# First pair of heads: the products of q and k ahead of the decay's matmuls, and the scaled decay sum behind the low part

## The reference, cut to what matters

```
scores = scale * q @ k.T                         # 32 heads of 576 x 64
cum    = cumsum(log(clip(f, 1e-4, 1)))           # one row of 576 for each head
decay  = cum[:, None] - cum[None, :]
scores = where(causal, -1e9, scores + decay)
attn   = softmax(scores);  y = attn @ v
x      = y of all heads, 2304 tokens x 512
h      = relu(x @ w_in)**2 @ w_out               # 512 -> 2048 -> 512
out    = the same with a quadratic-then-linear gate and a second pair of weights
```

## Time and profile before

| | |
|---|---|
| median of 3 runs | 948.94 us (948.78 to 949.65) |
| the profiled execution | 948.56 us |
| its span, first to last instruction | 946.7 us |
| TensorE busy | 938.7 us, 99% |
| VectorE, ScalarE, GpSimd busy | 65%, 68%, 18% |
| granted clock of TensorE | 1.00 throughout |

### The profile page before, as it was taken

The page is one execution under the profiler, slowest core; times in us unless marked ns, Lnnn a source line. Parts: engine busy times, 40 slices in busy tenths (PEclk is TensorE's granted clock), DMA queues, the critical chain, the costliest instruction groups (busy, mean ns, idle before and its releaser), DMA issues.

```text
span 946.7 us, 16672 instructions
## 1 busy us (share of the span) xinstructions
PE 938.7 (99%) x5554; PEld 865.6 (91%) x5554; DVE 613.5 (65%) x1279; ACT 642.2 (68%) x1342; POOL 167.8 (18%) x217
## 2 busy tenths in 40 slices
PE   8999999999999999999999999999999999999998
PEld 8999999989999999999999999898989888888897
DVE  7888888786666543446353588878766565755454
ACT  7888888886667655557564587666766566756564
POOL 7877999910000000000000000000000000000000
PEclk9999999999999999999999999999999999999999
DMA  6546555075557525252525144646545434364401
GB/s 217 168 152 181 162 190 159 24 245 176 191 187 290 200 101 187 114 197 104 200 102 201 45 153 141 239 133 262 228 179 193 174 132 169 130 229 143 165 24 68
DMA packets 61942, 155.13 MB, mean 164 GB/s; under 512 B 4624, under 2 KB 28688, under 8 KB 61872
## 3 DMA queue, kind: packets, MB, share of 16 engines
q1 hardware_dynamic: 61872, 154.23, 46.4%
HBM read 120.06 MB, written 34.15 MB: 163 GB/s over the span
## 4 chain that ended last, share of the span: by engine, by line
PE 96%; POOL 2%; issue 1%; ACT 1%; DVE 0%; POOLq 0%; ACTq 0%; DVEq 0%
PE banks L1469 37%; PE banks L1515 21%; PE banks L1507 14%; PE banks L1509 7%; PE banks L1413 6%; PE banks L1358 5%; PE banks L1368 4%; PE banks L1426 1%; PE banks L1384 1%; POOL wi_raw L780 1%; PE banks L1417 0%; PE banks L1409 0%; ACT pr L868 0%; POOL qk L692 0%; POOL xs L835 0%
## 5 line engine op out<-in xcount | busy, mean ns | idle before, releaser
L1469 PE MATMUL banks<-xs,wi_hi 128*128 128x384 f32 x1344 | 342.4, 335 | 1.4 <-ACT s_tile L942 0.7
L1469 PEld LDWEIGHTS banks<-xs,wi_hi 128*128 128x128 f32 x1344 | 235.2, 188 | 22.0 <-issue 1.9
L1469 PE MATMUL banks<-xs,wi_lo 128*128 128x384 f32 x672 | 224.7, 334 | 0.0
L1515 PE MATMUL banks<-wo_hi,gs 128*128 128x512 f32 x576 | 202.3, 393 | 0.0
L1507 PE MATMUL banks<-gs,wo_hi 128*128 128x512 f32 x384 | 141.7, 391 | 0.3 <-issue 0.3
L966 ACT ACTIVATE gs<-h_tile 128x384 fp32r<-128x384 f32 x192 | 100.7, 525 | 52.7 <-DVE h_tile L1214 50.0
L1469 PEld LDWEIGHTS banks<-xs,wi_lo 128*128 128x128 f32 x672 | 126.2, 188 | 0.0
L1515 PEld LDWEIGHTS banks<-wo_hi,gs 128*128 128x128 f32 x576 | 108.1, 188 | 18.8 <-DVE gs L1219 0.2
L942 ACT ACTIVATE s_tile<-banks 128x384 f32<-128x384 f32 x144 | 70.1, 487 | 76.3 <-PE banks L1469 76.1
L1515 PE MATMUL banks<-wo_lo,gs 128*128 128x512 f32 x288 | 113.7, 395 | 0.0
L1219 DVE TENSOR_TENSOR gs<-h_tile,gs 128x384 fp32r<-128x384 f32 x192 | 106.3, 554 | 7.0 <-ACT gs L966 6.1
(11 more groups left out here) (112 smaller groups left out, 1465.7 us busy)
## 6 DMA issues: line engine op xcount, KB each, us to landing
wi_hi<-kept_weights SPq DMA_DIRECT2D x32, 896.0 KB, 5.7
wi_lo<-kept_weights SPq DMA_DIRECT2D x32, 896.0 KB, 7.9
wo_raw<-moe_w_out_dram SPq DMA_DIRECT2D x48, 512.0 KB, 3.9
kept_weights<-wi_hi SPq DMA_DIRECT2D x16, 896.0 KB, 6.3
kept_weights<-wi_lo SPq DMA_DIRECT2D x16, 896.0 KB, 8.1
qk_raw<-qk_dram SPq DMA_DIRECT2D x15, 608.0 KB, 6.3
wi_raw<-moe_w_in_dram SPq DMA_DIRECT2D x32, 256.0 KB, 7.7
cb<-cum_scratch SPq DMA_DIRECT2D x30, 256.0 KB, 4.2
```

What stands on the lines that cost most here:

```text
L1469: last = mm(ps, w[a][:, W_OF[i], t * P:(t + 1) * P], xs[i][:, b, t, :], start=(i in (0, 1, 2, 5) and t == a == b == 0), stop=(i in (0, 3, ...
L1515: last = mm(banks[:, t, n0:n1], gs[:, q % 2, jj, a, t * P:(t + 1) * P], w[b][:, jj, n0:n1], start=(fresh and a == b == 0), stop=(done and ...
```

## The change

Three things. In the first pair, each tile's products now come first and its decay matmuls behind them (for tile 0 all six products, then four decay matmuls). With them TensorE's waits part: ahead of the products it waits for `first_lo` alone, and for `pick_ready` and `cum_lo` ahead of the first decay matmul. And GpSimd's L758 waits for `cum_lo`, VectorE's low part, where it waited for `cum_ready`, the sum itself.

```diff
@@ gpsimd
-            pool.wait_ge(cum_ready, 1)
+            pool.wait_ge(cum_lo, 1)
             nc.gpsimd.tensor_scalar(cum8[0:HEADS, :], cum[0:HEADS, :], -1.0 / SCALE, 0.0, ALU.mult, ALU.add)\
                 .then_inc(cum_scaled, 1)
@@ tensor: scores
                 if start and n == 0:
-                    pe.wait_ge(pick_ready, 3)
-                    pe.wait_ge(cum_lo, 1)
                     pe.wait_ge(first_lo, 1)
...
                     for n0 in range(0, WIDTH[u], half):
                         n1 = n0 + half
-                        if start:
-
-                            of = pick_tail if h == 2 else pick
-                            for part in range(2):
-                                mm(score_ps(u, WIDTH[u])[:, n0:n1], of[rows, :], cum_parts[part][rows, n0:n1],
-                                   start=(part == 0), stop=False)
                         for t, (a, b) in enumerate(((0, 0), (1, 0), (0, 1))):
                             last = mm(score_ps(u, WIDTH[u])[:, n0:n1], qk2[rows, par, a, i * P:(i + 1) * P],
                                       qk2[rows, par, b, QW + n0:QW + n1],
-                                      start=(t == 0 and not start), stop=(t == 2))
+                                      start=(t == 0), stop=(t == 2 and not start))
+                    if start:
+                        if n == 0:
+                            pe.wait_ge(pick_ready, 3)
+                            pe.wait_ge(cum_lo, 1)
+                        of = pick_tail if h == 2 else pick
+                        for n0 in range(0, WIDTH[u], half):
+                            for part in range(2):
+                                last = mm(score_ps(u, WIDTH[u])[:, n0:n0 + half], of[rows, :],
+                                          cum_parts[part][rows, n0:n0 + half], start=False, stop=(part == 1))
                     last.then_inc(scores_ready, 1)
```

## The result

The changed kernel takes 952.49 us (median of 7 executions, 951.54 to 955.31), before 948.94 (948.78 to 949.65); the ratio is 1.0041, 95% interval 1.0031 to 1.0050. It is slower by 3.6 us, more than the 1.9 us that the forecast took as the least that can be told from no change, and beyond the forecast's range of 949.1 to 951.3.

A forecast was written before the change was run, and what follows sets the result against it. TensorE, busy 938.7 of 946.7 us, was taken as the bound, waiting for GpSimd at 28.40. Terms 0 + 1.29 on the profiled 948.56 gave 949.85, hence a median of 950.2, range 949.1 to 951.3.

The forecast's parts named there:

- L758 and the queue: GpSimd's L758 ends 1.29 us later, behind VectorE's second L1069; the store and loads on SP's queue move with it.
- Part one: TensorE's first pair, products first: front 0.65 us earlier at best, lost on VectorE and the wait for GpSimd; 0 us.
- rival (b): Pair 2's decay loads, 1.3 us behind q and k, share the DMA engines: landing up to 1.1 us later, 951.3; 6%.
- q and k ... land at 20.27: SP's load of pair 2's q and k, issued at 13.97, lands at 20.27; GpSimd's stretch starts at 20.6.
- No term for the clock: TensorE idles 1.6 us or more before L1409; the sum adds nothing for a lower clock, 1.00 across an earlier 0.86.
- rival (c): TensorE's clock falls to 1.2 GHz behind the longer idle stretch; two us of work at that level give +3.3, 952.2; 3%.

The follow-up runs named there:

- the two remedies: Changed kernel plus loads of pair 2's decay held until VectorE's first maximum of pair 1, and 16 unused transposes in TensorE's idle stretch: 950.22 us, 1.0011.
- the change again: The changed kernel rerun with nothing altered, for the spread between executions: 952.06 us, traced execution 951.82.
- experiment 1: Changed kernel with L758 waiting for the sum as before, so only the products-first order differs from the kernel before: 949.31 us, ratio 1.0009.
- the hold: SP holds the loads of pair 2's decay until VectorE's first maximum of pair 1: changed kernel 950.03 us, with 16 unused transposes too 950.22.
- the load ahead: SP loads pair 2's q and k before pair 1's v: kernel before 948.31 us, products first alone 948.81, changed kernel 950.78.

## Why the prediction was wrong

The direction and the path were right, the size was not: +3.55 us in place of +1.29. Two terms were missing from the sum, a longer landing and the clock.

- **L758 and the queue: right.** Forecast: L1073 0.73 long, L758 ending at 9.04 behind the second L1069, q and k issued at 13.97. Measured 0.76, 9.10 and 14.04. L758 is recorded as 1.04 long but ends 0.52 after L1069's end at 8.58: turns again. By the rule of the Trainium skill (SBUF — State Buffer, "SBUF: two separate sides") L758 had to stand behind the whole instruction that came first, and the trace agrees. With the two remedies in, and products first, +1.33 is left.
- **Part one at 0 us: right as a sum, wrong in its surroundings.** The front was 1.1 us ahead, not 0.65: the products started at 7.31, as soon as `first_lo` was there. (The forecast had them wait for the warm-up's end at 7.80. In this trace it ended at 6.41; in the change again it is recorded to 7.74, and the products start at 7.49 all the same, since ends of matmuls are modelled.) It was lost where forecast, on VectorE's first tile with a mask (19.34, 1.77 us of waiting). What the forecast missed is that an earlier front can do harm: it sends the loads of pair 2's decay sooner (room 0.8, and not the 1.3 of rival (b)) and, with TensorE early and GpSimd late, makes the idle stretch longer (1.52 in experiment 1). By experiment 1's timing that harm is small.
- **"q and k ... land at 20.27": this step failed.** It kept the landing at 6.3 us. It was 6.7, 7.4 and 9.0 in the three traces of the change. The five traces with 3 us of room or more, with q and k in their old place, have 6.3 to 6.8; the six with less, 6.7 to 9.3. Rival (b) had this at 6%, with up to 1.1 us, and dismissed it because cbt had landed after q and k before. In the change the first load of cbt, issued behind q and k, landed ahead of them (14.82 + 6.1 = 20.9, against 14.04 + 9.0 = 23.0). The Trainium skill (DMA: Bandwidth & Descriptors, "Queues, rings and completion order") says that completion isn't in order per issuing engine; the trace agrees with that.
- **No term for the clock (rival (c), 3%): this step failed too, and it was the larger.** The forecast saw that TensorE would idle 1.6 us or more, and took one idle stretch of 0.86 us at a clock of 1.00, and the want of any row with the lower level, as evidence that the clock would stay up. Of the 14 traces, nine have an idle stretch of 1.5 us or more ahead of the product with v; the clock fell in eight of them, for 1.5 to 1.6 us in seven and 2.8 in one, and in none of the five with a shorter one. In all 14 executions of the change it was 0.998 or less. Rival (c)'s price of +3.3, 952.2, is near the median of 952.49 in part by luck: it has 2 us for the clock and nothing for the landing, where the runs have 1.5 to 1.6 and 0.4 or more.

Usual execution of the change: 1.3 (late L758) + 0.5 (longer landing, an estimate; 0.4 and 1.1 in its two usual traces) + 1.5 (clock) = 3.3 us, against 3.3 to 3.6 measured.

**What stays open.** Why the landing differs between executions of one program (6.7 to 9.0 with the same issue times within 0.1 us and 0.2 in the room) isn't shown. That the loads of cbt and cb are the cause isn't shown either: it rests on the hold, 0.4 us between two medians that scatter can make, and on two groups of landings that overlap (6.8 and 6.7). The room doesn't set the landing by itself: with the load ahead, it was 8.1 with 3.3 us of room and 6.8 with 1.5. A rival stands untested: pair 3's q and k, 608 KB, also go out later when the loads are held. In the six traces with less room they were issued at 18.15 to 18.50, ahead of the landing of pair 2's; in the five with more, at 18.95 to 21.51, at the landing or behind it. And it isn't known why 2.04 us of idle time left the clock alone in one trace and 1.52 didn't in another.

## What to carry to other kernels

A wait that GpSimd shares with nobody can still be the head of a long path: follow what its output releases, store, reload and next load, up to the busiest engine, before calling its engine idle. When a change opens an idle stretch on a TensorE that was at full clock, count the clock as a cost of its own (here 1.5 us on a delay of 1.8, behind stretches from 1.52 us up), and read the spread of the executions: two clusters show it. And don't carry a load's time to land over from one trace as a constant: here it went from 6.3 to as much as 9.3 us with nothing added ahead of it in its queue.

## What the runs showed that had not been expected

Sixteen transposes whose results nobody reads made the changed kernel 1.4 us faster. The landing of one 608 KB load ranged from 6.3 to 9.3 us with the same bytes ahead of it. The 30 transposes of the warm-up took 6.26 us in one trace and 4.87 in another, since their change of pace came anywhere between 4.4 and 7.4 us; two traces of the same program differ in this too (6.26 and 5.02 for the kernel before). And one execution of the kernel before, of 75 beside these experiments, was at 951.65 us with a clock of 0.998: it has no trace, so its idle stretch isn't known.
